# Packing two half-width passes into one: a tile of two batches in a fused attention and MLP kernel

## The chip, the cores and the metric

The kernel runs on one NeuronCore of a Trainium2 chip. The metric is the device time of one execution in microseconds (us), the median of several executions. Of the core's engines, TensorE (PE in the profile; its weight loads are listed as PEld), VectorE (DVE), ScalarE (ACT), GpSimd (POOL) and SyncE (SP, which here issues nearly all the DMAs) matter.

## The reference

```python
def _attn_ref(q, k, v):                      # q, k, v: (2 batches, 8 heads, 576, 64)
    ...                                      # rotary embedding of q and k
    scores = scale * np.matmul(q_rot, k_rot.transpose(0, 1, 3, 2))
    scores = scores - np.max(scores, axis=-1, keepdims=True)
    attn = np.exp(scores)
    attn = attn / (np.sum(attn, axis=-1, keepdims=True) + 1e-09)
    return np.matmul(attn, v).astype(np.float32)

def _moe_ref(x, w_in, w_out):                # x: (1152, 512), w_in: (512, 2048), w_out: (2048, 512)
    h = x @ w_in
    g = h * (1.0 / (1.0 + np.exp(-h)))
    return (g @ w_out).astype(np.float32)
```

The attention's output goes through `_moe_ref`, and its result through a second layer of the same size whose activation is ELU. All of it is float32.

## The kernel before

**Precision.** Every operand of a product is split in two: `hi`, the value rounded to TensorE's fp32r, and `lo`, the rest. A product is made of three passes over the array: hi times lo, hi times hi, lo times hi.

**Chunks and heads.** The 1152 tokens (two batches of 576) are worked on in three chunks of 384 columns (`CT`). Chunk 0 is tokens 0 to 383 of batch 0, chunk 2 is tokens 192 to 575 of batch 1, and chunk 1 holds the last 192 tokens of batch 0 and the first 192 of batch 1: its middle tile of 128 queries has 64 of each. A chunk has 8 heads, so heads are numbered 0 to 23 (`i`), and each head has three tiles of 128 queries (`QN`), numbered `n = 3 i + t`.

**Attention of a tile.** `score_tile` makes the scores of 128 queries against 576 keys in two halves of 288 columns. The 128 rows of the contraction hold 64 features twice: `q_one` has q_hi in both halves of the partitions, against `k_st`, which has k_hi in one and k_lo in the other; `q_two` has q_lo in one half and zeros in the other. So a tile of one batch takes 2 passes a half, 4 in all. The tile of two batches (chunk 1, t = 1) takes 4 passes a half, 8 in all: two for each batch, with queries of the other batch as zero columns (`PADS`). `max_tile` (DVE) and `exp_tile` (ACT) follow, then `transpose_tile` and `transpose_end` on PE turn the probabilities so that keys are on the partitions: four blocks of 128 keys and one last block (`END_BANK`), and `probs_hi`, `probs_lo`, `end_hi`, `end_lo` split them into `pt_hi`, `pt_lo` and `pt_end`. `value_products` (L879, L881) multiplies them with `v_st`, in which v_hi and v_lo stand side by side as 128 columns, so the result has v_hi's share on 64 rows and v_lo's on the other 64, and `copy_out_lo` (ACT, L475) and `add_outputs` (DVE, L650) add the two halves. In chunk 1 each of the two batches has its own keys and values, so `value_products` makes two sets of 9 products of 192 columns.

**MLP.** A chunk's two layers are 64 units (`hidden_unit`, `output_unit`), each 12 products of 384 columns (L914). A unit needs one block of weights, 128 x 512, which SP loads (`load_unit`, L235), ACT rounds (`weight_hi`, L489) and POOL subtracts (`weight_lo`, L331).

**The order.** All engines run lists written out by hand. Chunk 0's attention (heads 0 to 7) runs alone; then chunk c's 64 units run with chunk c+1's attention between them, 8 units to a head: unit n goes with head `i = 8 + n // 8` at step `j = n % 8`. `tile_at` says at which steps a tile is transposed (the last tile of the head before at j = 0, tile 0 at j = 3, tile 1 at j = 5; in the last head of a chunk at 2, 4 and 6); the next tile is scored right behind it. In chunks 1 and 2 the last block of keys of tiles 0 and 1 is transposed with tile 1, that of tile 2 with tile 2. The value products of a head stand in the next head at j = 2, `add_outputs` at j = 4 (3 in a chunk's last head). At j = 7, SP calls `place` (L217 to L223), which copies the split queries and keys of head i + 2 from `q_raw` and `k_raw` into `q_one`, `q_two` and `k_st`: five DMAs, with the weight loads in the same queue.

## Time and profile before

| | |
|---|---|
| median of 3 runs | 562.35 us (562.2 to 563.34) |
| profiled execution: its time | 561.98 us |
| profiled execution: its span in the trace | 560.2 us |
| PE busy in the span | 536.2 us (96%) |
| DVE, ACT, POOL busy | 279.0, 344.6, 347.5 us |
| granted TensorE clock | full speed in all slices |
| chunk 0's attention / its MLP with chunk 1's attention / chunk 1's MLP with chunk 2's attention / chunk 2's MLP | about 0 to 63 / to 250 / to 427 / to 560 us |

The span is the time between the first and the last instruction of the trace; 1.8 us of the execution lie around it. Products overlap in TensorE's pipeline: one of 384 columns is listed as 335 ns long though the next starts 174 ns behind it, so a product's price is read from the distance of starts, or from the chain of work, which merges products in a row and gives their time together. PE's time is nearly all of the span between 63 and 560 us.

### The profile page before, as it was taken

What the parts mean: (1) busy time and instruction counts of PE and PEld (TensorE: products, weight loads), DVE (VectorE), ACT (ScalarE), POOL (GpSimd) and SP (SyncE); (2) the same over time, 40 slices, a digit from 0 to 9 for tenths busy, and PEclk for the clock granted to TensorE, in tenths of its full rate; (3) what the DMA queues carried; (4) which work ended last, traced back from release to release, by engine and by line L of the source; (5) the groups of instructions that cost most, each with busy time, mean ns of one, the idle gap of its engine ahead of it and who ended that gap; (6) DMA issues with size and microseconds to landing.
All of it is one profiled execution on the core that took longest, in us unless ns stands there. A gap on an engine that the chain in (4) does not pass through costs nothing.

```text
span 560.2 us, 9272 instructions
## 1 busy us (share of the span) xinstructions
PE 536.2 (96%) x3308; PEld 529.0 (94%) x3308; DVE 279.0 (50%) x503; ACT 344.6 (62%) x726; POOL 347.5 (62%) x287
## 2 busy tenths in 40 slices
PE   1888889999999999999999999999999999999997
PEld 1777889999999999999999999999999999999997
DVE  5788755633258762336563237884334440057400
ACT  4899777755467765557775457775555663366531
POOL 6989989659646565645655654454544666656652
PEclk9999999999999999999999999999999999999999
DMA  8676735365254353344434442334333434334440
GB/s 332 199 219 187 204 102 179 103 198 160 95 166 138 99 165 124 113 116 152 124 108 142 117 117 91 116 105 136 111 108 110 131 129 134 123 124 131 130 144 29
DMA packets 43229, 77.16 MB, mean 138 GB/s; under 512 B 5296, under 2 KB 12848, under 8 KB 43184
## 3 DMA queue, kind: packets, MB, share of 16 engines
q1 hardware_dynamic: 41456, 74.21, 42.8%
q10 hardware_dynamic: 1728, 2.36, 1.1%
q8 instruction: 27, 0.44, 0.3%
q14 instruction: 18, 0.15, 0.1%
HBM read 63.57 MB, written 2.36 MB: 118 GB/s over the span
## 4 chain that ended last, share of the span: by engine, by line
PE 92%; ACT 3%; DVE 3%; issue 1%; DMA 1%; SPq 0%; ACTq 0%; DVEq 0%
PE banks L914 71%; PE banks L879 6%; PE banks L849 5%; PE banks L833 3%; PE banks L835 3%; PE banks L858 1%; ACT prob L449 1%; DVE neg_max L619 1%; PE banks L881 1%; DMA k_raw<-k 1%; PE banks L892 1%; DVE head_out L656 0%; ACT q_raw L434 0%; ACT k_st L419 0%; DVE pt_lo L626 0%
## 5 line engine op out<-in xcount | busy, mean ns | idle before, releaser
L331 POOL TENSOR_TENSOR w_lo<-w_raw,w_hi 128x512 fp32r<-128x512 f32 x192 | 246.8, 1288 | 194.8 <-ACT w_hi L489 194.5
L489 ACT CAST w_hi<-w_raw 128x512 fp32r<-128x512 f32 x189 | 117.7, 624 | 45.1 <-PE banks L914 41.2
L914 PE MATMUL banks<-x_lo,w_hi 128*128 128x384 f32 x384 | 129.8, 338 | 1.4 <-DVE x_lo L661 0.7
L914 PE MATMUL banks<-g_lo,w_hi 128*128 128x384 f32 x384 | 129.3, 337 | 0.0
L914 PE MATMUL banks<-g_hi,w_lo 128*128 128x384 f32 x384 | 128.7, 335 | 0.0
L914 PE MATMUL banks<-x_hi,w_lo 128*128 128x384 f32 x384 | 128.7, 335 | 0.0
L914 PE MATMUL banks<-x_hi,w_hi 128*128 128x384 f32 x384 | 128.5, 335 | 0.0
L914 PE MATMUL banks<-g_hi,w_hi 128*128 128x384 f32 x384 | 128.5, 335 | 0.0
L619 DVE TENSOR_REDUCE neg_max<-banks 128x1 f32<-128x576 f32 x72 | 54.3, 754 | 70.8 <-PE banks L835 69.4
L501 ACT ACTIVATE act_buf<-banks 128x384 f32<-128x384 f32 x96 | 47.2, 492 | 58.0 <-PE banks L914 57.7
L914 PEld LDWEIGHTS banks<-x_lo,w_hi 128*128 128x128 f32 x384 | 72.1, 188 | 3.1 <-DVE x_lo L661 1.6
L914 PEld LDWEIGHTS banks<-x_hi,w_hi 128*128 128x128 f32 x384 | 72.2, 188 | 0.0
L914 PEld LDWEIGHTS banks<-g_hi,w_hi 128*128 128x128 f32 x384 | 72.2, 188 | 0.0
L914 PEld LDWEIGHTS banks<-g_lo,w_hi 128*128 128x128 f32 x384 | 72.1, 188 | 0.0
L914 PEld LDWEIGHTS banks<-x_hi,w_lo 128*128 128x128 f32 x384 | 72.1, 188 | 0.0
L914 PEld LDWEIGHTS banks<-g_hi,w_lo 128*128 128x128 f32 x384 | 72.1, 188 | 0.0
L449 ACT ACTIVATE prob<-banks,neg_max 128x576 f32<-128x576 f32 x72 | 53.6, 744 | 29.3 <-DVE neg_max L619 28.2
L833 PE MATMUL banks<-k_st,q_one 128*128 128x288 f32 x160 | 52.1, 342 | 10.5 <-DVE q_two L675 10.5
L701 DVE SCALAR_TENSOR_TENSOR g_lo<-banks,g_hi 128x384 fp32r<-128x384 f32 x96 | 52.9, 551 | 5.9 <-ACT g_hi L508 5.9
L849 PE MATMUL banks<-ident,prob 128*128 128x128 f32 x288 | 45.2, 281 | 9.2 <-ACT prob L449 8.9
L457 ACT CAST pt_hi<-banks 128x512 fp32r<-128x512 f32 x60 | 35.4, 590 | 29.7 <-PE banks L849 27.9
L685 DVE SCALAR_TENSOR_TENSOR banks<-act_buf,banks 128x384 f32<-128x384 f32 x48 | 27.0, 562 | 47.9 <-ACT act_buf L501 47.9
(75 smaller groups left out, 723.2 us busy)
## 6 DMA issues: line engine op xcount, KB each, us to landing
w_raw<-w SPq DMA_DIRECT2D x192, 256.0 KB, 2.6
q_raw<-q SPq DMA_DIRECT2D x11, 384.0 KB, 3.1
q_one<-q_raw SPq DMA_DIRECT2D x44, 96.0 KB, 2.6
k_raw<-k SPq DMA_DIRECT2D x7, 576.0 KB, 4.6
k_st<-k_raw SPq DMA_DIRECT2D x28, 144.0 KB, 2.5
v_raw<-v SPq DMA_DIRECT2D x8, 320.0 KB, 3.0
out<-act_buf ACTq DMA_DIRECT2D x12, 192.0 KB, 2.5
q_two<-q_raw SPq DMA_DIRECT2D x22, 96.0 KB, 2.3
```

Source lines behind the costliest of these rows:

```text
L331: nc.gpsimd.tensor_tensor(w_st[LO][:, slot, :], w_raw[:, slot, :], w_st[HI][:, slot, :].bitcast(F32), ALU.subtract).then_inc(w_lo_done, 1)
L449: nc.scalar.activation(halves(prob[:, n % 3, :]), scores(n), ACT.Exp, bias=neg_max[:, n % 2:n % 2 + 1], accum_out=row_sum[:, i // 2 % 2, t ...
L457: nc.scalar.copy(pt[HI][buffer_of(i)][:, :, t * P:(t + 1) * P], probs_t(n)).then_inc(pt_hi_done, 1)
L489: nc.scalar.copy(w_st[HI][:, slot, :], w_raw[:, slot, :]).then_inc(w_hi_done, 1)
L501: nc.scalar.activation(act_buf[:, ft % 2, :], mlp(USES * c + 20 * layer + ft), func, scale=scale) \
L619: nc.vector.tensor_reduce(neg_max[:, n % 2:n % 2 + 1], scores(n), AXES.XY, ALU.max, negate=True) \
L685: nc.vector.scalar_tensor_tensor(bank, buf, 1.0, bank, ALU.add, ALU.mult).then_inc(h_read, 1)
L701: nc.vector.scalar_tensor_tensor(g[LO][:, ft, :], mlp(USES * c + 20 * layer + ft), (0.5, 1.0)[layer], g[HI][:, ft, :].bitcast(F32), ALU.mu ...
L833: nc.tensor.matmul(scores(n)[:, a, :], q_one[par][:, col:col + P], k_st[:, slot, keys], start=m == 0, stop=False)
L849: last = nc.tensor.transpose(probs_t(n)[:, m, :], prob[:, n % 3, m * P:(m + 1) * P], ident[:, :])
L879: nc.tensor.matmul(pv_out[:, cols], v_st[:, slot, m, :], pt[part][buf][:, m, cols], start=m == 0 and part == LO, stop=False)
L914: last = nc.tensor.matmul(dst, w_st[wp][:, slot, m * P:(m + 1) * P], src[xp][:, tile, :], start=start and n == 0, stop=stop and n == 2)
```

## The change

- **Scores of the tile of two batches.** A new tile `k_both` holds k_hi of one batch on 64 partitions and k_hi of the other on the other 64. `q_two` holds the 64 queries of one batch on one half of the partitions and the 64 of the other batch on the other, with zeros elsewhere (`BOTH`, `BOTH_OTHER`). One pass then makes q_lo times k_hi for both batches: 3 passes a half, 6 in all. `q_two` is placed by three DMAs instead of one for each head of chunk 1, and `k_both` is filled by two DMAs a head (`place_both`, at j = 7; for head 8 in `place`). Four small memsets on DVE set the zeros; two on POOL go.
- **Value products of chunk 1.** `pt_hi` and `pt_lo` are one tile `pt`, so one product reads 192 columns of the high and 192 of the low probabilities beside each other, 384 in all. The results of the two batches go to two banks, `END_BANK` and `PV_BANK`, each with the high part in columns 0 to 191 and the low part in 192 to 383. A batch takes 4 products of 384 columns and 1 of 192: 10 a head, before 18.
- **Adding up.** ACT copies the high part of one half of the rows as before; DVE adds two parts instead of one, the second addition waiting for the first (`out_part_added`).
- **Last keys.** In chunks 1 and 2 the last blocks of all three tiles are transposed together with the head's last tile. In chunk 1 the first of them also waits for `out_added` of the head before, since `END_BANK` holds that head's products until then.

```diff
+BOTH, BOTH_OTHER = slice(128, 192), slice(192, 256)
...
+        k_both = sb("k_both", [P, S], F32R)
...
-        pt_tile = [sb("pt_hi", [P, 4 * CT], F32R), sb("pt_lo", [P, 4 * CT], F32R)]
+        pt_tile = sb("pt", [P, 2, 4 * CT], F32R)
...
-                sp.dma_start(placed(q_two[par], i, rows).bitcast(F32), q_lo).then_inc(ready, 16)
+                if i // H == 1:
+                    q_lo = q_raw[r % 2][rows, 0, :]
+                    sp.dma_start(ends_of(q_two[par][rows, 0:CT]).bitcast(F32), ends_of(q_lo)).then_inc(ready, 16)
+                    sp.dma_start(q_two[par][rows, BOTH].bitcast(F32), q_lo[:, P:P + D]).then_inc(ready, 16)
+                    sp.dma_start(q_two[par][others, BOTH_OTHER].bitcast(F32), q_lo[:, P + D:2 * P]) \
+                        .then_inc(ready, 16)
...
+            def place_both(i):
...
+                sp.wait_ge(scored, QN * (i - 1) + 2)
+                sp.wait_ge(placed_in[par], placed_count(i // 2))
+                sp.dma_start(k_both[rows, :].bitcast(F32), k_st[rows, i % SLOTS, :].bitcast(F32)) \
+                    .then_inc(both_in, 16)
+                sp.dma_start(k_both[others, :].bitcast(F32), k_st[rows, i % H, :].bitcast(F32)) \
+                    .then_inc(both_in, 16)
...
+                if j == 7 and H < i + 1 < 2 * H:
+                    place_both(i + 1)
...
+                if i // H == 1:
+                    nc.vector.tensor_tensor(halves(dst), pv_parts(rows, LO), halves(dst), ALU.add) \
+                        .then_inc(out_part_added, 1)
+                    dve.wait_ge(out_part_added, i - H + 1)
+                    nc.vector.tensor_tensor(halves(dst), pv_parts(rows, HI), halves(dst), ALU.add) \
+                        .then_inc(out_added, 1)
...
+                if c == 1 and t == 1:
+                    pe.wait_ge(both_in, 32 * (i - H + 1))
+                    ones = ((P, own), (2 * P, other))
...
+                    if c == 1 and t == 1:
+                        keys_two = k_both[:, keys]
...
+                if t == 0 and H < i <= 2 * H:
+                    pe.wait_ge(out_added, i)
...
+                    for bank, slot in ((END_BANK, own), (PV_BANK, other)):
+                        col = (bank - END_BANK) * 192
+                        for m in range(4):
+                            nc.tensor.matmul(banks[:, bank, 0:CT], v_st[:, slot, m, :],
+                                             pt_tile[:, :, m * CT + col:m * CT + col + 192], start=m == 0, stop=False)
+                        last = nc.tensor.matmul(banks[:, bank, HI * 192:HI * 192 + 192], v_st[:, slot, 4, :],
+                                                pt_end[buf][:, col:col + 192], start=False, stop=True)
...
-                            if tile == 1:
-                                transpose_end(m - 1)
-                            if tile:
-                                transpose_end(m)
+                            if m % QN == QN - 1:
+                                for e in range(m - 2, m + 1):
+                                    transpose_end(e)
```

On PE, the value products of head 8 (beside unit 10), before and then now; a row is an instruction, with the size of its output and, in brackets, the semaphores it waits for:

```order
L879 MATMUL banks<-pt_lo,v_st 128x192 [waits v_lo_done,out_scaled,end_lo_done,pt_lo_done]
L879 MATMUL banks<-pt_hi,v_st 128x192
L879 MATMUL banks<-pt_lo,v_st 128x192
L879 MATMUL banks<-pt_hi,v_st 128x192
L879 MATMUL banks<-pt_lo,v_st 128x192
L879 MATMUL banks<-pt_hi,v_st 128x192
L879 MATMUL banks<-pt_lo,v_st 128x192
L879 MATMUL banks<-pt_hi,v_st 128x192
L881 MATMUL banks<-pt_end,v_st 128x192
```

```order
L945 MATMUL banks<-pt,v_st 128x384 [waits v_lo_done,out_scaled,end_lo_done,pt_lo_done]
L945 MATMUL banks<-pt,v_st 128x384 x3
L947 MATMUL banks<-pt_end,v_st 128x192
L945 MATMUL banks<-pt,v_st 128x384 x4
L947 MATMUL banks<-pt_end,v_st 128x192
```

The nine rows before are one batch's, and nine alike follow; now five products stand for them, and the second batch's five follow in the same place.

On PE, the score passes of the tile of two batches of head 9, behind its tile 0's transposes, before and now:

```order
L849 MATMUL banks<-ident,prob 128x128 x3
L833 MATMUL banks<-k_st,q_one 128x288 [waits pads_zero,exp_done]
L835 MATMUL banks<-k_st,q_two 128x288
L833 MATMUL banks<-k_st,q_one 128x288
L835 MATMUL banks<-k_st,q_two 128x288
L833 MATMUL banks<-k_st,q_one 128x288
L835 MATMUL banks<-k_st,q_two 128x288
L833 MATMUL banks<-k_st,q_one 128x288
L835 MATMUL banks<-k_st,q_two 128x288
```

```order
L916 MATMUL banks<-ident,prob 128x128 x3
L896 MATMUL banks<-k_st,q_one 128x288 [waits both_zero,both_in,pads_zero,exp_done]
L896 MATMUL banks<-k_st,q_one 128x288
L902 MATMUL banks<-k_both,q_two 128x288
L896 MATMUL banks<-k_st,q_one 128x288 x2
L902 MATMUL banks<-k_both,q_two 128x288
```

Two of the four passes with `q_two` are gone, and the first pass waits for the DMAs of `k_both` as well.

On SP, the queue between two weight loads at the end of head 8 (j = 7), before and now:

```order
L217 DMA q_one<-q_raw 64x2x192 [waits scored,q_lo_done]
L218 DMA q_one<-q_raw 64x2x192
L219 DMA q_two<-q_raw 64x2x192
L222 DMA k_st<-k_raw 64x576 [waits k_lo_done]
L223 DMA k_st<-k_raw 64x576
L235 DMA w_raw<-w 128x512 [waits w_lo_done] x8
```

```order
L256 DMA k_both<-k_st 64x576 [waits placed_in_b,scored]
L258 DMA k_both<-k_st 64x576
L232 DMA q_one<-q_raw 64x2x192 [waits scored,q_lo_done]
L233 DMA q_one<-q_raw 64x2x192
L236 DMA q_two<-q_raw 64x2x128
L237 DMA q_two<-q_raw 64x64
L238 DMA q_two<-q_raw 64x64
L244 DMA k_st<-k_raw 64x576 [waits k_lo_done]
L245 DMA k_st<-k_raw 64x576
L271 DMA w_raw<-w 128x512 [waits w_lo_done] x8
```

Nine DMAs instead of five stand in front of the next weight load.

## Rows read from the trace of the kernel before

**Rows 1.** The page's part 1, busy time, and part 4, the chain by engine.

```profile
PE 536.2 (96%) x3308; PEld 529.0 (94%) x3308; DVE 279.0 (50%) x503; ACT 344.6 (62%) x726; POOL 347.5 (62%) x287
...
PE 92%; ACT 3%; DVE 3%; issue 1%; DMA 1%; SPq 0%; ACTq 0%; DVEq 0%
```

**Rows 2.** Chain in order of time, chunk 1's attention: start us, us, what.

```profile
93.47 0.87 PE banks L879 x8
...
95.45 2.13 PE banks L914 x12
...
103.68 0.22 PE banks L858 x2
...
120.51 0.13 PE banks L833
...
121.57 0.53 PE banks L914 x3
```

**Rows 3.** The same view in chunk 2's attention, value products of 384 columns.

```profile
274.52 1.41 PE banks L879 x8
```

**Rows 4.** PE's waits between 64 and 250 us: total, times, longest.

```profile
PE banks L914 <- DVE g_lo L701: 0.7, 2, 0.5
```

**Rows 5.** Chain in order of time, start of chunk 0's MLP.

```profile
76.06 0.52 ACT act_buf L501
...
77.82 0.47 DVE g_lo L701
```

**Rows 6.** DVE's timeline: start, us, line, operation, idle before and its releaser.

```profile
103.81 0.56 DVE L685 SCALAR_TENSOR_TENSOR banks<-act_buf,banks 128x384 f32<-128x384 f32 x1 [0.60 <-ACT act_buf L501]
...
171.07 0.56 DVE L650 TENSOR_TENSOR head_out<-banks,head_out 64x384 f32<-64x384 f32 x1
...
174.93 0.55 DVE L689 SCALAR_TENSOR_TENSOR act_buf<-act_buf,banks 128x384 f32<-128x384 f32 x1 [0.35 <-ACT act_buf L501]
...
249.23 0.56 DVE L650 TENSOR_TENSOR head_out<-banks,head_out 64x384 f32<-64x384 f32 x1 [3.24 <-ACT head_out L475]
250.66 0.55 DVE L656 TENSOR_TENSOR head_out<-head_out,banks 128x384 f32<-128x384 f32 x1 [0.88 <-PE banks L892]
```

**Rows 7.** SP's timeline at the end of head 9.

```profile
109.76 0.63 SPq L217 DMA_DIRECT2D q_one<-q_raw  x1
...
112.39 1.53 SPq L223 DMA_DIRECT2D k_st<-k_raw  x1
115.84 0.33 SPq L206 DMA_DIRECT2D q_raw<-q  x1
...
116.70 6.68 SPq L235 DMA_DIRECT2D w_raw<-w  x5
```

**Rows 8.** Line L235 between 116.5 and 117.1 us: one weight load.

```profile
DMA to landing us min/median/max: 4.3/4.3/4.3
```

**Rows 9.** ACT's timeline behind it.

```profile
121.04 0.62 ACT L489 CAST w_hi<-w_raw 128x512 fp32r<-128x512 f32 x1
122.40 0.74 ACT L449 ACTIVATE prob<-banks,neg_max 128x576 f32<-128x576 f32 x1 [0.74 <-DVE neg_max L619]
```

**Rows 10.** Chain in order of time: the transposes that need that tile.

```profile
125.74 0.44 PE banks L849 x4
```

**Rows 11.** SP's timeline before and at the start of chunk 0's MLP.

```profile
57.12 0.58 SPq L223 DMA_DIRECT2D k_st<-k_raw  x1
...
65.44 1.37 SPq L235 DMA_DIRECT2D w_raw<-w  x3
```

**Rows 12.** Line L223 between 57 and 58 us.

```profile
DMA to landing us min/median/max: 2.5/2.5/2.5
```

**Rows 13.** Line L235 between 65 and 67 us: three weight loads.

```profile
DMA to landing us min/median/max: 5.4/5.5/6.4
```

**Rows 14.** PE's timeline: the first score pass of head 8.

```profile
60.83 0.38 PE L833 MATMUL banks<-k_st,q_one 128*128 128x288 f32 x1
```

**Rows 15.** ACT's timeline: the cast of the first of those three weights.

```profile
73.30 0.61 ACT L489 CAST w_hi<-w_raw 128x512 fp32r<-128x512 f32 x1
```

More of the change, by code:

```diff
@@ L77, in build @@
         ident = sb("ident", [P, P])
-        pt = [[pt_tile[part][:, :].rearrange("p (t n) -> p t n", t=4), g[part][:, 0:4, :]] for part in (HI, LO)]
+        pt = [[pt_tile[:, part, :].rearrange("p (t n) -> p t n", t=4), g[part][:, 0:4, :]] for part in (HI, LO)]
         pt_end = [pt_end_tile[:, :], g[HI][:, 4, :]]
@@ L86, in build, with pv_parts @@
         pv_out = banks[:, PV_BANK, 0:CT]
+        def pv_parts(rows, part):
+            return banks[rows, END_BANK:END_BANK + 2, part * 192:part * 192 + 192]
         def inv_rows(p):
@@ L474, in copy_out_lo @@
                     act.wait_ge(x_lo_done, p - 1)
-                nc.scalar.copy(head_out[p % 2][rows_of[par], :], pv_out[other_rows_of[par], :]) \
-                    .then_inc(out_lo_copied, 1)
+                dst, others = head_out[p % 2][rows_of[par], :], other_rows_of[par]
+                if i // H == 1:
+                    nc.scalar.copy(halves(dst), pv_parts(others, HI)).then_inc(out_lo_copied, 1)
+                else:
+                    nc.scalar.copy(dst, pv_out[others, :]).then_inc(out_lo_copied, 1)
             def output_hi(p):
@@ L648, in add_outputs @@
                 p, rows = i // 2, rows_of[i % 2]
+                dst = head_out[p % 2][rows, :]
                 dve.wait_ge(out_lo_copied, i + 1)
-                nc.vector.tensor_tensor(head_out[p % 2][rows, :], pv_out[rows, :], head_out[p % 2][rows, :], ALU.add) \
-                    .then_inc(out_added, 1)
+                if i // H == 1:
+                    nc.vector.tensor_tensor(halves(dst), pv_parts(rows, LO), halves(dst), ALU.add) \
[3 more added lines that the diff above has]
+                        .then_inc(out_added, 1)
+                else:
+                    nc.vector.tensor_tensor(dst, pv_out[rows, :], dst, ALU.add).then_inc(out_added, 1)
             def scale_outputs(p):
@@ L792, in _ @@
                     continue
+                if n < 2:
+                    dve.wait_ge(scored, QN * (7 + n))
+                    nc.vector.memset(q_two[n][rows_of[n], BOTH_OTHER].bitcast(F32), 0.0).then_inc(both_zero, 1)
+                if i == 2 * H - 1 and j in (3, 7):
+                    par = j // 4
+                    dve.wait_ge(scored, QN * (2 * H - 2 + par) + 2)
+                    nc.vector.memset(q_two[par][other_rows_of[par], BOTH_OTHER].bitcast(F32), 0.0) \
+                        .then_inc(both_zero, 1)
                 if i % H == H - 1:
```

45 lines of the change are left out of this document (28 added, 17 removed).

## The prediction, made before the changed kernel was timed

> **What bounds the kernel now.** I read the page first: PE is busy for 96% of the span and holds 92% of the chain that ended last [rows 1]. So time taken from PE's list is time taken from the kernel, as long as PE stays the bound where it is taken. The change touches chunk 1's attention, which runs between 63 and 250 us beside the MLP of chunk 0, so the second view is PE's waits in that stretch. The only kind that matters there is a wait of 0.7 us in all for DVE's `g_lo`, in two places [rows 4], both at the start of the chunk's MLP, where the chain goes through ACT and DVE [rows 5]. From about 79 us to the end of the MLP of chunk 0 the chain is PE alone. The third view is that chain in order of time, which gives the price of each group of products in place.
>
> **The value products of chunk 1.** Before, a head makes 18 products of 192 columns. The chain has them from 93.47 us to the next unit's first at 95.45: 1.98 us, or 0.11 each (the first eight take 0.87) [rows 2]. Now a head makes 8 of 384 columns and 2 of 192. The nearest row for 384 columns with the same stationary operand is chunk 2's: eight take 1.41 us, 0.176 each [rows 3]. So 1.41 + 2 x 0.11 = 1.63, which is 0.35 less a head, 2.8 us for eight heads. The number of columns streamed is the same (18 x 192 = 8 x 384 + 2 x 192 = 3456); what is saved is that a product of 192 columns costs 0.11 us where its half of a 384-column product costs 0.088. Bounds: the new operand is read in two pieces of 192 a row, 1536 columns apart. No row here has such a read on PE. If each piece cost what a product of 192 costs, eight would take 16 x 0.11 = 1.76, and the saving would be 1.98 - 1.98 = 0. Above, 0.088 per half for all eighteen gives 1.58 and a saving of 0.4 a head. I take 0.35, since the piece is not an instruction, and what costs 0.11 lies between instructions.
>
> The Trainium skill weighs against this term: "TensorE: Matmul & The Clock Gate", section "Back-to-back issue gap", gives an isolated product N/2.4 + 2.5 ns. An estimate by it is 82.5 ns for 192 columns and 162.5 for 384, and a head would go from 1.49 to 1.47 us: no gain. The trace contradicts it for this kernel, 0.11 us for 192 columns with a new stationary operand each time [rows 2]; the same page's section "LDWEIGHTS (loading the stationary operand)" gives 128 columns / 1.2 = 107 ns, and that agrees.
>
> **The scores of the tile of two batches.** Eight passes take from 120.51 to 121.57 us, 0.13 each [rows 2]. Two go, 0.26 a head. In head 8 this stands at 74 to 75 us, where PE then waits for `g_lo` anyway, and that time is set by ACT and DVE [rows 4, 5]; there I count nothing. Seven heads give 1.85 us.
>
> **The last keys.** The same transposes stand in another place: two of them take 0.22 us behind tile 1 [rows 2], and now they take that behind tile 2. Their number is the same, and so is PE's time: 0. `exp_tile` of the next head waits for them, but it also waits for scores that stand behind them on PE. The bank's new user: the first of these transposes waits for `out_added`, and the additions stand at j = 4 of the same head's steps, four units of 2.1 us [rows 2] ahead. Nothing, and the bound is nothing too while the addition isn't later than that.
>
> **The second addition on DVE.** One more operation of 0.56 us a head [rows 6]. Beside hidden units DVE's results free PE's banks, so this can reach PE. In head 9 the addition stands in front of an operation that has 0.60 us of idle time before it [rows 6]: covered. In head 12 it stands at 171.07 us, nothing is idle behind it until 174.93, where 0.35 is [rows 6]; the results in between come up to 0.56 us later, and the PE units that need them start, by the units' places in the list, a fraction of a microsecond after that. Head 13 is alike. In heads 10, 11 and 14 it stands beside output units, which leave DVE free. At the end of the chunk it lies on the way from head 15's products to the next chunk's x: but there DVE waits 0.88 us for PE's `spread_sums` after the addition [rows 6], which covers 0.56. So 0 is taken, and 3 x 0.56 = 1.7 us is the bound.
>
> **SP's queue.** Before, `place` issues five DMAs, and four steps lie between 109.76 and 112.39 us, 0.66 each [rows 7]. Now it issues seven for heads up to 15, and `place_both` two in front of it: four more, 2.6 us, ahead of the weight loads, and in odd heads ahead of the loads of the next q and k too, which wait for the placed data to land (115.84 us). The next weight load is issued at 116.70 [rows 7] and lands 4.3 us later [rows 8], at 121.0; ACT casts it at 121.04 [rows 9], so it has nothing to spare. With 2.6 us more ACT stands still until 123.6, and the exponential behind it, at 122.40 before [rows 9], starts at about 124.2 and ends at 124.95; PE wants it transposed at 125.74 [rows 10]. So 0.8 us is left, and the cover for the added delay is 3.4 us in all. The weight itself is used by PE several us later still. The same happens at the ends of heads 11 and 13. Value taken: 0; below zero it can't go, because an added DMA frees nothing.
>
> At the start two more things hang on the queue. The last key DMA of head 8 is issued at 57.12 [rows 11] and lands 2.5 us later [rows 12]; two more DMAs in front make that 60.9, and PE wants it at 60.83 [rows 14]: 0.1 us at most. And three weight loads are issued from 65.44 us [rows 11], land after 5.4 [rows 13], and the first is cast at 73.30 [rows 15], on the path through ACT: 2.5 us to spare. Six DMAs are added in front, 3.9 us at 0.66 each, of which SP can put some into its waits for the scores. Bounds 0 and 1.4 us; I take 0, as SP waits there.
>
> The small memsets (DVE four more, POOL two fewer) stand where their engine waits for something else: nothing. ACT's copy has as many elements as before.
>
> **Sum.** 2.8 + 1.85 = 4.65 us off the profiled execution's own 561.98 us gives 557.3. The median of the runs is 562.35, 0.37 above the profiled one, so the same saving puts the median at **557.7 us**.
>
> **Rivals.**
> - *The additions reach PE* [rows 6]. If the bank that the second addition delays is the one PE wants next in heads 9, 12 and 13, up to 1.7 us come back: 558.3 to 559.4. For it speaks that DVE is without idle time behind 171.07; against it the 0.60 and 0.35 us.
> - *The two-piece operand costs as two products* [rows 2, 3]. Then only the scores gain: 562.35 - 1.85 = 560.5. The Trainium skill's gap formula named above comes to the same time by another way. Against both stands the 0.11 us of the trace, which belongs to the instruction.
> - *The queue is a little slower than its steps.* The last key DMA's issue took 1.53 us instead of 0.66 [rows 7], so SP can be held. If two of the four added DMAs are held so, the delay is 4.4 us, 1.0 more than the cover, at three heads: 557.7 + 3 = 560.7.
> - *The queue turns the gain into a loss.* If all four are held for 1.53 us, the delay is 6.1 us, 2.7 over the cover at three heads, 8.1 us in all: 565.8, slower than before. It decides from 1.55 us over the cover at each of the three places, a delay of about 5 us. Pieces of 64 columns (256 bytes a row) among the added DMAs speak for it; that weight loads have about 5 us between cast and use on PE speaks against, and that the DMA engines are not full in this stretch.
>
> The Trainium skill, "DMA: Bandwidth & Descriptors", names 512 bytes as the least size for full rate. No row of before has a smaller piece to check it.
>
> **How the numbers follow.** The forecast has a chance of 0.72, with a range of its own from 557.1 to 558.5 (the upper bound of the products' saving, 0.05 x 8, and head 8's 0.26 below; the start's stalls above). The additions 0.09, the two-piece operand 0.05, the slow queue 0.08, a loss by the queue 0.04, and 0.02 is left for a larger gain than summed. The range of 557.0 to 560.3 takes in the forecast, the additions and part of the others. A measurement can tell about 0.2%, 1.1 us, from no change: faster than 561.2 is then 0.91, within 0.05, slower 0.04.
>
> **What would show it.** In the chain of the changed kernel, a head's value products in chunk 1 should take about 1.63 us from the first to the next unit, with eight of 384 columns at 0.176 each; the middle tile's scores about 0.80. PE's waits between 79 and 250 us should stay near nothing. ACT should show a new wait of about 2.6 us for a weight's DMA in front of L489's counterpart once in each odd head, without a wait of PE for `prob` behind it. If PE waits for `prob`, the queue's cover was misjudged; if PE waits for `g_lo` in heads 9, 12 or 13, the additions' was; if products of 384 columns stand 0.2 us or more apart, the operand's price was.

## The result, and the profile after

| | before | changed |
|---|---|---|
| median of 6 runs each, taken together | 562.95 us (562.2 to 563.62) | 558.09 us (557.16 to 558.62) |
| profiled execution: its time, its span | 561.98, 560.2 us | 557.37, 555.6 us |

The ratio is 0.9912, with a 95% interval from 0.9899 to 0.9926: faster by 0.9%. The forecast of 557.7 us lies 0.4 below the median, and the 557.3 that it gave for the profiled execution lies 0.1 below what that took. PE is still the bound. The page's part 1 and its chain by engine, changed kernel (beside [rows 1]):

```profile
PE 530.8 (96%) x3228; PEld 523.0 (94%) x3228; DVE 282.6 (51%) x515; ACT 343.8 (62%) x726; POOL 347.1 (62%) x285
...
PE 86%; DMA 4%; SPq 3%; ACT 3%; DVE 2%; issue 2%; POOL 0%; ACTq 0%; DVEq 0%
```

PE has 80 instructions and 5.4 us of busy time fewer, and DVE has 3.6 us more. The chain now goes through SP's queue and a DMA (SPq and DMA, 7%), which it hardly did before.

The chain in order of time, head 9 of the changed kernel (start us, us, what; the counterpart of [rows 2]):

```profile
93.83 0.71 PE banks L945 x4
94.54 0.09 PE banks L947
94.63 0.73 PE banks L945 x4
95.36 0.09 PE banks L947
95.45 2.10 PE banks L986 x12
...
97.99 0.27 PE banks L896 x2
98.26 0.13 PE banks L902
...
98.79 4.19 PE banks L986 x24
```

The value products take 95.45 - 93.83 = 1.62 us, against 1.98 before, and the six score passes 98.79 - 97.99 = 0.80 us.

Where the time went is read from PE's timeline by stretches: from the first product of a head's first unit to the first product of the next head's. A stretch holds eight units and one head's attention; head 15's also holds its own value products. All values in us, from the profiled executions:

| kernel | start to unit 0 | head 8 | 9 | 10 | 11 | 12 | 13 | 14 | 15 | chunk 1's MLP | the rest |
|---|---|---|---|---|---|---|---|---|---|---|---|
| before | 64.55 | 24.56 | 22.49 | 22.84 | 22.49 | 22.84 | 22.49 | 22.84 | 24.50 | 173.56 | 137.02 |
| changed | 64.62 | 24.86 | 21.86 | 22.47 | 21.86 | 22.16 | 21.83 | 22.16 | 23.46 | 173.30 | 137.00 |

Heads 9 and 11 to 15 gain 0.63 to 0.68 each (head 15, with two sets of value products, 1.04). Head 10 gains 0.37 only, head 8 loses 0.30, and chunk 1's MLP, beside chunk 2's attention, gains 0.26. Where nothing holds PE, these stretches repeat to 0.03 us from one kernel to another. The first column doesn't: it lies between 64.1 and 66.0 us over the kernels below, and it begins with the first loads of q and k, which no edit touches. So differences of some tenths are read here from the stretches, and the medians, which contain that first column, are the check.

**Head 10's 0.3 us.** The view is SP's timeline at the end of head 9 in the changed kernel (the counterpart of [rows 7]):

```profile
109.26 0.47 SPq L256 DMA_DIRECT2D k_both<-k_st  x1
...
111.78 1.66 SPq L236 DMA_DIRECT2D q_two<-q_raw  x1
...
115.41 0.60 SPq L245 DMA_DIRECT2D k_st<-k_raw  x1
117.90 0.33 SPq L221 DMA_DIRECT2D q_raw<-q  x1
...
118.76 1.84 SPq L271 DMA_DIRECT2D w_raw<-w  x4
```

Nine DMAs stand ahead of the weight now. From the first of them to the weight's issue it takes 118.76 - 109.26 = 9.50 us, before 116.70 - 109.76 = 6.94: 2.56 more, and the 2.6 of the prediction is right. The weight then takes 4.7 us to land, where it took 4.3 before [rows 8]. One DMA is held (1.66 us instead of about 0.6), as one was before (1.53). The load of the next q (L221) waits for the placed data to land and is issued at 117.90 only, 1.9 us after L245's issue ended, and the weight stands behind it. ACT's timeline shows what follows (counterpart of [rows 9]; the bracket is the idle time before and its releaser):

```profile
119.86 0.59 ACT L494 CAST pt<-banks 128x512 fp32r<-128x512 f32 x1 [2.07 <-PE banks L916]
123.48 0.62 ACT L529 CAST w_hi<-w_raw 128x512 fp32r<-128x512 f32 x1 [3.03 <-DMA w_raw<-w]
124.00 0.74 ACT L486 ACTIVATE prob<-banks,neg_max 128x576 f32<-128x576 f32 x1
```

ACT waits 3.03 us for the weight, and the exponential stands behind the cast. The chain joins them to PE's transposes:

```profile
118.76 4.70 DMA w_raw<-w
...
124.64 0.20 ACT prob L486
...
124.88 0.66 PE banks L916 x4
```

PE stood 0.31 us there: its stretch is 22.47 us where every like one is 22.16.

**Head 8's 0.3 us.** The chain at the start of chunk 0's MLP:

```profile
67.96 5.66 DMA w_raw<-w
73.64 0.49 ACT w_hi L529
```

The first of three weight loads is issued at 67.96 instead of 65.44 us [rows 11], 2.5 later, and its cast starts at 73.64 instead of 73.30 [rows 15], now released by the load.

### The profile page after: what moved, and what is told of

It is laid out like the page before. It is cut to its first block, busy times and chain, and to the rows that moved or that the text cites. A ratio compares the mean times of both kernels' runs of the same rounds, so it can differ in the third digit from the quotient of the medians.

```text
span 555.6 us, 9179 instructions
## 1 busy us (share of the span) xinstructions
PE 530.8 (96%) x3228; PEld 523.0 (94%) x3228; DVE 282.6 (51%) x515; ACT 343.8 (62%) x726; POOL 347.1 (62%) x285
## 4 chain that ended last, share of the span: by engine, by line
PE 86%; DMA 4%; SPq 3%; ACT 3%; DVE 2%; issue 2%; POOL 0%; ACTq 0%; DVEq 0%
PE banks L986 69%; PE banks L916 5%; PE banks L896 3%; PE banks L952 3%; PE banks L902 3%; DMA w_raw<-w 2%; PE banks L945 2%; PE banks L927 1%; ACT prob L486 1%; DMA k_st<-k_raw 1%; DMA k_raw<-k 1%; DVE neg_max L659 1%; PE banks L964 1%; SPq L236 1%; PE banks L954 0%
## 5 line engine op out<-in xcount | busy, mean ns | idle before, releaser
L896 PE MATMUL banks<-k_st,q_one 128*128 128x288 f32 x160 | 49.9, 342 | 11.1 <-DVE q_two L722 11.0
L494 ACT CAST pt<-banks 128x512 fp32r<-128x512 f32 x60 | 35.4, 590 | 28.7 <-PE banks L916 26.9
```

What stands on the lines that cost most here:

```text
L494: nc.scalar.copy(pt[HI][buffer_of(i)][:, :, t * P:(t + 1) * P], probs_t(n)).then_inc(pt_hi_done, 1)
L896: nc.tensor.matmul(scores(n)[:, a, :], q_one[par][:, col:col + P], k_st[:, slot, keys], start=m == 0, stop=False)
```

## The experiments

Each edit is to the changed kernel. The table has their stretches in us, read as above. The excess of head 10 is what its stretch takes more than that of head 12 of the same kernel, or of head 12 of the changed kernel where both are held.

| kernel | median us | ratio to before, 95% | head 8 | 9 | 10 | 11 | 12 | 13 | 14 | 15 | chunk 1's MLP |
|---|---|---|---|---|---|---|---|---|---|---|---|
| scores only | 561.37 | 0.9984 (0.9975 to 0.9993) | 24.80 | 22.25 | 24.18 | 22.25 | 22.60 | 22.25 | 22.60 | 24.26 | 173.53 |
| values only | 558.71 | 0.9933 (0.9921 to 0.9945) | 24.56 | 22.10 | 22.40 | 22.07 | 22.40 | 22.07 | 22.40 | 23.70 | 173.28 |
| split products | 561.01 | 0.9977 (0.9965 to 0.9989) | 25.28 | 22.25 | 23.78 | 22.23 | 22.55 | 22.23 | 22.55 | 24.25 | 173.30 |
| one piece | 558.53 | 0.9931 (0.9919 to 0.9943) | 25.39 | 21.86 | 22.33 | 21.86 | 22.16 | 21.83 | 22.16 | 23.46 | 173.28 |
| last keys with tile 1 | 562.52 | 1.0006 (0.9995 to 1.0017) | 24.77 | 22.34 | 23.78 | 21.84 | 23.27 | 22.78 | 22.18 | 23.52 | 173.57 |
| two more operations | 563.44 | 1.0019 (1.0009 to 1.0028) | 24.86 | 23.05 | 24.39 | 21.85 | 23.24 | 23.06 | 22.16 | 23.46 | 173.52 |
| spread queue | 559.08 | 0.9942 (0.9930 to 0.9954) | 26.83 | 21.86 | 22.16 | 21.83 | 22.16 | 21.83 | 22.16 | 23.46 | 173.28 |
| four more DMAs | 564.59 | 1.0044 (1.0021 to 1.0066) | 25.05 | 23.87 | 24.27 | 21.86 | 24.09 | 21.83 | 23.47 | 23.46 | 173.29 |
| weights first, `k_both` early | 557.24 | 0.9911 (0.9898 to 0.9924) | 24.56 | 21.86 | 22.16 | 21.83 | 22.16 | 21.83 | 22.16 | 23.46 | 173.28 |
| weights first | 557.41 | 0.9908 (0.9895 to 0.9921) | 24.58 | 21.86 | 22.16 | 21.83 | 22.16 | 21.83 | 22.16 | 23.46 | 173.31 |
| four more, weights first | 558.95 | 0.9935 (0.9922 to 0.9948) | 24.58 | 23.55 | 22.18 | 21.83 | 22.16 | 22.38 | 22.16 | 23.46 | 173.31 |
| changed kernel again | 558.62 | 0.9932 (0.9919 to 0.9946) | 25.05 | 21.86 | 22.16 | 21.83 | 22.16 | 21.83 | 22.16 | 23.46 | 173.31 |

### The scores alone

The value products, their adding up and the last keys are put back as before; `q_two` and `k_both` stay.

> The scores' part of the change alone: k_both, the three pieces of q_two and the three passes a half, with the value products, additions and transposes of the last keys as before. If the gain is PE's products and the queue's cost belongs to the placing, 7 x 0.26 = 1.85 us are gained and about 0.6 given back (0.34 at the start of chunk 0's MLP, 0.24 in head 10): 1.3 us below before, so about 561.6 beside a before of 562.9, with ACT's wait of 3 us for a weight's DMA at the end of head 9. Rival: the whole gain comes from one part, and this one is either 0 or over 4 us below before.

Measured: heads 9 and 11 to 15 take 0.24 us less than before, 1.7 us for seven heads. All of the queue's DMAs are in this kernel, and in its profile they cost 1.6 at head 10 and 0.2 at head 8, all of that and a little more. ACT's and PE's waits between 64 and 250 us (us in total, times, longest):

```profile
ACT w_hi L529 <- DMA w_raw<-w: 5.7, 2, 4.3
...
PE banks L916 <- ACT prob L486: 1.4, 1, 1.4
```

The held DMA took 2.03 us in this run, and the weight behind it 5.8 us to land instead of 4.7. The scores' part is worth what was summed, and its queue takes back up to 1.6 at head 10. By the medians 0.9 us are left of the gain, so the other executions lose less there than the profiled one.

### The value products alone

`q_two`, `k_both` and the score passes are put back; products, additions and last keys stay changed.

> The value products' part alone: 10 products a head, two additions, the last keys transposed with a head's last tile; scores, q_two and the queue of DMAs as before. By the sum: 8 x 0.35 = 2.8 us below before, so about 560.1, no wait of ACT for a weight's DMA over 0.1 us. With e1 it should add up to what the change measured (4.9 us by the medians). Rival: the queue costs nothing and the values give less, 1.5 us or so below before.

Measured: 3.6 us off the stretches. Each head gains 0.39 to 0.44 instead of 0.35 (head 15's stretch, with two sets, 0.80), and chunk 1's MLP, in which no value product changes, gains 0.28. ACT waits 0.2 us for a weight in all and PE never for `prob`, and head 8 takes 24.56 us as before. So what is given back in the changed kernel comes with the scores' DMAs. By the ratios the two parts, 0.9 and 3.8 us, add up to 4.7, beside 4.9 for the change.

### The same products, not joined

Banks and operands as in the changed kernel, but the high and the low probabilities in products of their own, 18 a head.

```diff
-                        for m in range(4):
-                            nc.tensor.matmul(banks[:, bank, 0:CT], v_st[:, slot, m, :],
-                                             pt_tile[:, :, m * CT + col:m * CT + col + 192], start=m == 0, stop=False)
...
+                        for part in (HI, LO):
+                            out = banks[:, bank, part * 192:part * 192 + 192]
+                            for m in range(4):
+                                last = nc.tensor.matmul(out, v_st[:, slot, m, :],
+                                                        pt_tile[:, part, m * CT + col:m * CT + col + 192],
```

> The changed kernel with each value product of 384 columns split again into one of 192 high and one of 192 low probabilities, in the same banks: 18 products a head for 10, all else as changed. If an instruction of 192 columns costs 0.11 us, a head's products go from 1.62 to 1.98 us and the time rises by 8 x 0.36 = 2.9 us, to about 561. Rival: the streamed columns alone count (18 x 192 either way), then it rises by 0.2 us at most.

The chain in order of time, head 9:

```profile
94.60 0.42 PE banks L947 x4
95.02 0.11 PE banks L951
...
96.58 1.44 PE banks L990 x8
```

It is 1.98 us again, 0.11 a product, and the stretches rise by 0.39 (head 15's by 0.79). This alone tells what joining is worth: 0.39 us a head, 3.1 us in all, with nothing else changed. By the gap formula N/2.4 + 2.5 of the Trainium skill ("TensorE: Matmul & The Clock Gate", section "Back-to-back issue gap") it would have been 0.02; the run decides against that formula for these products, which each bring a new stationary operand. The section says itself that the formula holds for an isolated product and counts too little at small N.

### The operand in one piece

Each joined product reads 384 neighbouring columns of the high probabilities, so the low probabilities' share is left out; the number and the size of the products are the same.

```diff
-                                             pt_tile[:, :, m * CT + col:m * CT + col + 192], start=m == 0, stop=False)
+                                             pt_tile[:, HI, m * CT:m * CT + CT], start=m == 0, stop=False)
```

> The changed kernel with the 384 columns of a value product read in one piece (the high probabilities of all 384 tokens of the chunk) instead of two pieces 1536 columns apart: the low probabilities' share is left out and wrong columns are used, so only its time counts. If two pieces cost nothing, the same within 0.2 us, 1.62 us for a head's products. Rival: the second piece costs some 10 ns a product (1.44 us for eight against 1.41 in chunk 2): 0.2 us less a kernel at most; if more, the sum's price was wrong.

The chain in head 9:

```profile
95.75 0.71 PE banks L945 x4
96.46 0.09 PE banks L947
```

These are the changed kernel's own prices, and its stretches are the same in head 9 and from head 11 on. (Heads 8 and 10 differ by what the queue costs, see below.) Reading the operand in two pieces, 1536 columns apart, costs nothing.

### The last keys with tile 1, as before

```diff
-                            if m % QN == QN - 1:
-                                for e in range(m - 2, m + 1):
-                                    transpose_end(e)
+                            if tile == 1:
+                                transpose_end(m - 1)
+                            if tile:
+                                transpose_end(m)
```

> The changed kernel with the last keys of tiles 0 and 1 transposed with tile 1 again, where they stood before. They wait for out_added, whose addition stands one unit earlier on DVE. By the ends of the second addition in the changed kernel's trace and the starts of tile 1's transposes, PE would wait 0.3, 1.7, 0.9 and 0.7 us in heads 9, 10, 12 and 13: 3.6 us above the changed kernel, about 561.7. Rival: the place of these transposes makes no difference, since PE's work is the same: 558.1.

PE's waits between 64 and 250 us:

```profile
PE banks L927 <- DVE head_out L695: 3.3, 4, 1.4
```

The four waits are 0.3 us in head 9, 1.4 in head 10, 0.9 in head 12 and 0.7 in head 13, as expected but for head 10's 1.7, and the kernel is at the time of before. Two things follow. The move of the last keys isn't a detail: `END_BANK` holds the value products of the head before until DVE's second addition, and with tile 1 the transposes want it too early. And chunk 1's MLP takes 173.57 again, 0.27 more than with the last keys together: the new place is worth 0.03 to 0.04 us a head by itself. It isn't the transposes that got cheaper. Added up from the starts of PE's products in that stretch, before and changed, the transposes of chunk 2's attention take 11.13 and 11.12 us and the score passes 13.99 and 14.22, while the distances between the products of the units come to 128.65 and 128.17 (128.65 again in this run). What shortens those distances stays open.

### Two more operations behind the first addition

```diff
-                    dve.wait_ge(out_part_added, i - H + 1)
+                    for again in range(2):
+                        dve.wait_ge(out_part_added, 3 * (i - H) + again + 1)
+                        nc.vector.tensor_tensor(dst, dst, dst, ALU.max).then_inc(out_part_added, 1)
+                    dve.wait_ge(out_part_added, 3 * (i - H) + 3)
```

> The changed kernel with two more DVE operations of the same shape (each the maximum of the partial sum with itself, so the result is the same) between the two additions of a head of chunk 1, 1.2 us more a head in a row. If DVE's cover beside hidden units is what the trace of the changed kernel shows (0.65, 0.26 and 0.30 us between g_lo and the unit that waits for it in heads 9, 12 and 13), PE waits about 0.5, 0.9 and 0.9 us there: 2.3 us above the changed kernel, 560.4. Rival: DVE is off the path altogether: 558.1.

DVE's timeline in head 9:

```profile
102.67 0.54 DVE L692 TENSOR_TENSOR head_out<-banks,head_out 64x384 f32<-64x384 f32 x1
103.25 1.70 DVE L696 TENSOR_TENSOR head_out<-head_out 64x384 f32<-64x384 f32 x2
104.98 0.55 DVE L698 TENSOR_TENSOR head_out<-banks,head_out 64x384 f32<-64x384 f32 x1
```

The same pair in heads 12 and 13:

```profile
173.15 1.15 DVE L696 TENSOR_TENSOR head_out<-head_out 64x384 f32<-64x384 f32 x2
...
196.22 1.23 DVE L696 TENSOR_TENSOR head_out<-head_out 64x384 f32<-64x384 f32 x2
```

The two operations took 1.70 us in head 9, more than meant, and 1.15 and 1.23 in heads 12 and 13. They move the second addition by 1.74, 1.18 and 1.26 us (the distance from the first addition's start to the second's, less the 0.57 to 0.60 of the changed kernel), and the stretches rise by 1.19, 1.08 and 1.23. So 0.55 us is covered in head 9, 0.10 in head 12 and 0.03 in head 13, less than the 0.65, 0.26 and 0.30 expected. The change's own second addition adds 0.6 us and moved no stretch: in heads 12 and 13 it fills what was free to within 0.1 us. Head 10 waits 1.4 us by another way, at `spread_sums`, which follows the additions, and 0.4 for `prob`, and chunk 1's MLP takes 0.22 more; the two operations also lie on the way to its x. The time rises by 5.4 us over the changed kernel, more than the expectation, which left out head 10 and chunk 1's MLP.

### `k_both` earlier, behind the weights at the start

```diff
-                if i == H:
-                    sp.dma_start(k_both[rows, :].bitcast(F32), k_raw[r % 2][rows, 1, :]).then_inc(both_in, 16)
-                    sp.dma_start(k_both[others, :].bitcast(F32), k_st[rows, 0, :].bitcast(F32)).then_inc(both_in, 16)
...
+            place_both(H)
...
-                if j == 7 and H < i + 1 < 2 * H:
+                if j == 5 and H < i + 1 < 2 * H:
```

> The changed kernel with the DMAs of k_both moved in SP's queue, from j = 7 in front of place to j = 5 of the same head, and for head 8 behind the three weight loads. If the queue's delay is what costs 0.34 us at the start and 0.24 us in head 10, both go: 0.5 us below the changed kernel, about 557.6 beside 558.1, and ACT's wait for a weight at the end of head 9 falls from 3.0 to about 1.7 us. Rival: the delay of placing q_two in three pieces is what counts, or neither: within 0.1 us of the changed kernel.

Head 10's excess is gone (22.16), and ACT's longest wait for a weight is 0.7 us. (The changed kernel's second profile, below, has 22.16 in head 10 too, so only ACT's wait tells what the move did.) At the start the edit was wrong, and the run says how a DMA fares behind three weight loads of 256 KB. The chain:

```profile
68.40 7.29 DMA k_both<-k_st
75.69 0.14 issue
75.82 0.69 PE banks L894 x2
```

It landed 7.29 us after SP took it up, and PE waited 2.0 us for it. Head 8's stretch is 2.0 above the changed kernel's, and that is why the median is above its too.

### Four more DMAs

`k_both` in six DMAs instead of two.

```diff
+                for third in range(3):
+                    cols = slice(third * 192, third * 192 + 192)
+                    sp.dma_start(k_both[rows, cols].bitcast(F32), k_st[rows, i % SLOTS, cols].bitcast(F32)) \
+                        .then_inc(both_in, 16)
+                    sp.dma_start(k_both[others, cols].bitcast(F32), k_st[rows, i % H, cols].bitcast(F32)) \
+                        .then_inc(both_in, 16)
```

> The changed kernel with each of the two DMAs that fill k_both cut in three of 192 columns: the same bytes, four more DMAs in SP's queue in front of place in heads 8 to 14. At 0.66 us each the queue is 2.6 us later. If the cover is 3.4 us as predicted, ACT's wait for a weight at the end of head 9 grows from 3.0 to 5.6 us and PE's for the exponential from 0.24 to about 2.8; with 0 to 1.9 us at the end of head 11 and 0.7 at 13, 3 to 5 us above the changed kernel: 561 to 563. Rival: the queue is hidden altogether and the 0.24 us has another cause: 558.1.

Waits between 64 and 250 us:

```profile
ACT w_hi L531 <- DMA w_raw<-w: 17.5, 7, 4.8
...
PE banks L918 <- ACT prob L488: 3.3, 4, 1.8
```

It is slower than before by 0.4%. Heads 9, 10, 12 and 14 rise by 2.01, 1.80, 1.93 and 1.31. ACT's wait in head 10 is 4.8 us and PE's excess 2.1, where 5.6 and 2.8 were expected. This was the rival that turns the gain into a loss, and its mechanism is real: 2.6 us more in the queue are enough. Head 9 shows that the end of an even head bites too, which the prediction didn't count.

### The order in the queue

```diff
                 if j == 7 and p + 1 < ITERS // 2:
                     place(p + 1, i % 2)
-                    if i % 2:
-                        if p + 3 < ITERS // 2:
-                            load_queries(p + 3)
-                        if p + 3 < 8:
-                            load_keys(p + 3)
                 if n + RING + AHEAD < ALL_UNITS:
                     load_unit(n + RING + AHEAD)
+                if i % 2 and j == 7:
+                    if p + 3 < ITERS // 2:
+                        load_queries(p + 3)
+                    if p + 3 < 8:
+                        load_keys(p + 3)
```

At the start the three weight loads go ahead of the last loads of q and k in the same way. Four kernels ran together: this order, with `k_both` at j = 5 as well; this order alone; this order with the four more DMAs; and the changed kernel again.

> The changed kernel with SP's list in another order: in an odd head's j = 7 the next weight load stands ahead of the loads of the next q and k instead of behind them, the same at the start (three weight loads ahead of the last q and k), and the two DMAs of k_both stand at j = 5 instead of j = 7. Nothing is left out. Theory (what is given back goes by SP's queue): the load behind head 9's placing is issued at about 115 us instead of 118.76, ACT waits for a weight less than 0.5 us in all between 64 and 250 us (4.7 in the changed kernel), the 0.3 us of PE's wait at the start of head 10 goes (24 units from head 8's end in 66.5 instead of 66.5 + 0.3), and the start gives back up to 0.3 us: 557.5 to 557.8, 0.3 to 0.6 below the changed kernel. Rival (the 0.3 us at head 10 comes from PE being early against DVE and ACT, not from the queue): ACT's wait for the weight goes, PE's wait of about 0.3 us stays, and the time is that of the changed kernel, 558.1.

> The same without the move of k_both: its two DMAs stay at j = 7. Theory: the weight's issue no longer waits for the placed data to land, so it comes about 2.7 us earlier (118.76 less the landing of 2.43 and the 0.3 of a load); ACT's wait at head 10 falls from 3.0 to about 0.4 us, under the cover of 2.8, and PE's stall of 0.3 us there goes: 557.5 to 557.8, the same as with k_both moved too. Rival (the wait for the landed data isn't what holds the weight, the number of DMAs ahead is): ACT's wait stays at 2 us or more and only moving k_both helps.

> The kernel with k_both placed by six DMAs instead of two, with the weight loads ahead of the loads of q and k as in the runs beside it. Without that order it took 564.6, with stalls of 1.8, 1.9 and 1.3 us at the starts of heads 10, 12 and 14 (behind the placing in an odd head, where q and k are loaded) and 2.0 at head 9 (behind the placing in an even head, where nothing else is loaded). Theory (order in SP's queue): the three go and the one at head 9 stays, 564.6 - 5.0 = 559.6, less 0.3 for the start, 559.3 to 560. Rival (so many DMAs in flight delay the weight whatever the order): the stalls stay, and the time is 563.5 or more.

> The changed kernel itself, beside the three reordered ones on the same chip, so that differences of 0.1% can be told: 558.1, with PE's wait of 0.3 us at the start of head 10 and ACT's of 3.0 us for the weight there.

(The 66.5 us in the first of these was added up wrongly: units 8 to 31 take 66.19 in the changed kernel and 65.85 where nothing holds PE.) SP's timeline with the order alone:

```profile
115.35 0.60 SPq L245 DMA_DIRECT2D k_st<-k_raw  x1
115.99 0.58 SPq L271 DMA_DIRECT2D w_raw<-w  x1
117.86 0.33 SPq L221 DMA_DIRECT2D q_raw<-q  x1
118.29 0.38 SPq L216 DMA_DIRECT2D k_raw<-k  x1
118.72 1.37 SPq L271 DMA_DIRECT2D w_raw<-w  x3
```

ACT's timeline of the same kernel, and then of the changed kernel's second profile:

```profile
120.54 0.59 ACT L495 CAST pt<-banks 128x512 fp32r<-128x512 f32 x1 [2.06 <-PE banks L917]
121.03 0.62 ACT L530 CAST w_hi<-w_raw 128x512 fp32r<-128x512 f32 x1
```

```profile
120.35 0.59 ACT L494 CAST pt<-banks 128x512 fp32r<-128x512 f32 x1 [2.06 <-PE banks L916]
123.54 0.62 ACT L529 CAST w_hi<-w_raw 128x512 fp32r<-128x512 f32 x1 [2.60 <-DMA w_raw<-w]
```

With the weight ahead of the loads that wait for landed data, ACT has no wait for a weight left between 64 and 250 us. The weight gains twice: it is issued 6.05 us behind the placing's first DMA instead of 9.50 or 9.04, and it lands in 2.9 us instead of 4.7. Head 8 is at 24.56 and 24.58 us, as before the change. The four more DMAs then cost nothing at heads 10, 12 and 14. Head 9 stays 1.69 over, and head 13 is 0.55 over, which it wasn't in the run without the order; both come behind an even head, where nothing stood to be reordered. So at the end of an odd head it isn't how many DMAs are in flight that hurts, it is that the weight stands behind the loads of q and k; at the end of an even head the number ahead of the weight still counts. The two reordered kernels have medians 1.4 and 1.2 us below the changed kernel's beside them; their stretches account for 0.5 (head 8). The rest isn't in the profiled executions, which took 557.27 and 557.78 us beside 557.57, and no trace shows where the others differ; the first 65 us alone vary by 1.9. Head 10's excess didn't occur in the changed kernel's second profile, so against that profile nothing is gained there. Both are better than the changed kernel and than before, by an amount near what can be measured; moving `k_both` as well adds nothing that shows.

## Why the prediction was right, point by point

- **Value products: right, slightly small.** 1.62 us measured for 1.63, a gain of 0.36 in the products, and 0.39 in the stretch when only the joining is undone. The 0.03 is in the unit behind them, 2.10 us instead of 2.13. In all that is 3.1 instead of 2.8. Both rival prices, the two pieces and the gap formula, fell by a run each.
- **Scores: right.** 0.24 a head for 0.26, 1.7 us for 1.85. Head 8's was put at nothing: with the weights first its stretch is 24.56, the same as before, though two passes are gone.
- **Last keys: the step that was mis-sized on the side of the gain.** It was put at 0, since the transposes are the same in number. Measured: 0.26 us in chunk 1's MLP, and about as much in chunk 0's, what is left of 3.6 when 3.1 and 0.26 are taken away. The transposes did stay at the same cost, as the prediction had it; the 0.26 lies in the distances between the units' products (128.17 us for 128.65), and why is open. That the bank's new user finds it free was right, but because of this move: with tile 1 it costs 3.3 us of waits.
- **Second addition: right, without much room.** Nothing showed in the changed kernel. Two more operations showed 1.1 to 1.2 us in each of heads 9, 12 and 13, the three that the prediction had named. In heads 12 and 13 they showed all but 0.10 and 0.03 of their length: the prediction could only guess at "a fraction of a microsecond" there, and that the addition just fitted is partly luck.
- **SP's queue at the end of head 9: the delay right, the cover 0.6 to 0.7 us too large.** The prediction gave a new wait of 2.6 us and 3.4 us of cover. The wait was 3.0 and 2.6 in two profiles of the changed kernel, and PE stood 0.3 and 0. The wait is made of two things: the time from the placing's first DMA to the weight's issue, and the weight's landing (all in us). Head 10's excess against ACT's wait gives the cover:

| kernel | first DMA to the weight's issue | landing | ACT's wait | excess | difference |
|---|---|---|---|---|---|
| before | 6.94 | 4.3 | 0 | 0 | |
| changed, second profile | 9.04 | 4.7 | 2.60 | 0.00 | |
| one piece | 9.59 | 4.5 | 2.89 | 0.17 | 2.72 |
| changed | 9.50 | 4.7 | 3.03 | 0.31 | 2.72 |
| split products | 9.06 | 6.4 | 3.93 | 1.23 | 2.70 |
| scores only | 9.90 | 5.8 | 4.33 | 1.58 | 2.75 |
| four more DMAs | 11.77 | 4.3 | 4.81 | 2.11 | 2.70 |
| weights first | 6.05 | 2.9 | 0 | 0.00 | |

  It is 2.7 us in all five. (In two more kernels PE waits for DVE in head 10 as well, so they don't give it.) With split products the queue was as short as in the changed kernel's second profile; there the landing of 6.4 us made the loss. Most of the cover that is missing can be named. PE's timeline has the transposes of head 10's tile 0 and tile 1, whose distance is the room that ACT has, before and then in the changed kernel's second profile:

```profile
119.91 0.60 PE L849 MATMUL banks<-ident,prob 128*128 128x128 f32 x4
125.58 0.60 PE L849 MATMUL banks<-ident,prob 128*128 128x128 f32 x4
```

```profile
119.72 0.60 PE L916 MATMUL banks<-ident,prob 128*128 128x128 f32 x4
125.14 0.60 PE L916 MATMUL banks<-ident,prob 128*128 128x128 f32 x4
```

  5.67 us became 5.42, because the two score passes that the change takes away stood between them: the gain itself took 0.25 of the cover. Another 0.16 is a reading: the chain starts that group at 125.74 [rows 10], the timeline at 125.58. The last 0.2 to 0.3 stay open.
- **SP's queue at the ends of heads 11 and 13: nothing lost, but not by the predicted way.** The prediction said that "the same happens" there, with a new wait of ACT of about 2.6 us in each. SP's timeline at the end of head 11, changed kernel:

```profile
160.53 0.33 SPq L221 DMA_DIRECT2D q_raw<-q  x1
160.91 1.49 SPq L271 DMA_DIRECT2D w_raw<-w  x3
```

  The load of the next keys (L216), which stands ahead of the weight at the end of head 9, is not there, and no DMA of the placing was held. The weight is issued 7.99 us behind the placing's first DMA and lands in 3.3; before it was 5.52 and 3.3, where head 9's was 6.94 and 4.3. ACT doesn't wait at all there, and 0.9 us at the end of head 13. So the weight had time to spare at these ends (at least 2.5 and about 1.4 us, by what its way grew less ACT's wait), which the prediction, reading head 9's alone, didn't see.
- **SP's queue at the start: the step that failed.** It was put at 0 with a bound of 1.4, on the ground that SP could issue some of the added DMAs while it waits for scores. That part was right, 2.5 us of delay instead of 3.9. But the cover was exactly 2.5, and the loads took 5.66 us. Head 8's stretch is 0.30 over before in the first profile and 0.49 in the second; over the eight kernels with the same start list it is 0.2 to 0.8 (24.77 to 25.39, for 24.56). In the first profile the two losses are alike; in the second this is the only one.
- **The sum.** Predicted 4.65. Measured in the profile: 3.1 + 0.5 + 1.7 = 5.3 gained, 0.3 at head 8 and 0.3 at head 10 given back, and 0.1 in the first stretch: 4.6, the difference of the two profiled executions. Part of the closeness is luck: a gain (the last keys) and losses (heads 8 and 10) which were all left out are nearly of one size.

Of the rivals, the slow queue and the queue's loss were near: with the same nine DMAs and one of them held, head 10 loses 0 to 1.6 us from profile to profile. The rivals looked for the spread in SP's issues alone. These differ by 0.9 us between the kernels with nine DMAs in a row; the landing of the weight behind them differs by 2.1 (4.3 to 6.4). And the loss stayed small because it arose at one head's end, not at three.

## What to carry to other kernels

Two products that share a stationary operand are worth joining wherever their distance is set by the instruction and not by the columns; the operand may lie in two pieces. A cover read from the trace before has to be reduced by what the change itself gains up to that point. And in a queue that carries both, put the load that something waits for ahead of the loads that wait for something: four more DMAs cost nothing at three places once the weight stood ahead of the loads that wait for landed data. A row read at one place of a repeated pattern holds for the others only if the same things stand there: heads 11 and 13 have no load of keys.

## What the hardware showed that was not expected

- A product of 192 columns costs 0.11 us in a row of its like and 0.09 between products of 384 columns (the rows of L947 above), at the same granted clock, full speed.
- At the end of head 9, SP holds one DMA of the placing for longer than the 0.6 us of the others: 1.53 us before, 0.91 to 2.03 in the eight kernels with nine DMAs in a row, and 1.36 and 1.27 in the two with thirteen. Which one it is changes from run to run (the fifth and the seventh in two profiles of the same kernel). At the end of head 11 none was held in the changed kernel. What holds it stays open.
- A weight load of 256 KB that stands behind the loads of the next q and k took 4.3 to 6.4 us to land at the end of head 9; ahead of them it took 2.8 to 2.9 in the three kernels with that order. Together with the held DMA this decides whether PE stands, beside a cover of 2.7 us.
- The pieces of 64 columns, 256 bytes a row, landed no later than others. The changed kernel's line L238 at the end of head 9:

```profile
DMA to landing us min/median/max: 1.8/1.8/1.8
```

  `k_st`'s rows of 2304 bytes, nine times the bytes, took 2.43 us in the same placing, by the chain. The Trainium skill, "DMA: Bandwidth & Descriptors", section "Why small descriptors are slow (HBM only)", says that transfers within SBUF don't suffer from small pieces. These rows don't contradict it, but 16 KB are too few to show a rate.
- The two added operations of DVE (64 x 384, both operands in SBUF) took 0.55 us each where GpSimd was idle and up to 1.53 where it wasn't. In head 9 the first starts at 103.25 us, while this subtraction runs on GpSimd until 103.95:

```profile
102.67 1.28 POOL L369 TENSOR_TENSOR w_lo<-w_raw,w_hi 128x512 fp32r<-128x512 f32 x1 [0.16 <-ACT w_hi L529]
```

  It ends at 104.36, 0.41 us behind it. The other stretched ones, at 128.23, 129.10, 150.22, 196.22, 216.65 and 238.06 us, end 0.41 or 0.42 us behind the end of a GpSimd operation too. The addition that starts at 102.67, with one operand in PSUM, isn't stretched (0.54 us).
